# Routing inside the delta rule's walk, late zeroing of the experts' tails, and a wait per output bank in the last layer

## The reference

```python
for t in range(S):                                   # delta rule, 8 heads of 48, S = 768
    y[:, :, t] = einsum('bhd,bhde->bhe', q[:, :, t], state)
    v_old = einsum('bhde,bhd->bhe', state, kt)
    state = state + bt * einsum('bhd,bhe->bhde', kt, vt - v_old)
...
e_idx = argmax(x @ w_gate, axis=1)                   # 8 experts, one for each token
gate_w = probs[arange(N), e_idx]                     # softmax of the logits
eom = 1.0 / (1.0 + exp(-(x @ w_output_gate)))
for e in range(E):
    h = maximum(x[mask] @ w1[e], 0.0)                # 384 -> 1024
    out[mask] = gate_w[mask, None] * eom[mask, e, None] * (h @ w2[e])
...
h = maximum(maximum(x @ w1, x @ w2), x @ w3)         # 384 -> 768, three times
return h @ w_out                                     # 768 -> 384
```

## Time and profile before

| | |
|---|---|
| median of three runs | 1154.94 us (1149.84 to 1159.45) |
| profiled execution | 1154.56 us |
| its span in the trace | 1152.8 us |
| TensorE busy | 1012.1 us (88%) |
| VectorE busy | 482.1 us (42%) |
| ScalarE busy | 366.7 us (32%) |
| GpSimd busy | 324.4 us (28%) |

### The profile page before, as it was taken

How to read it: one execution, slowest core, us unless ns; L and a number is a source line. 1 busy time by engine, 2 the same in 40 slices (tenths; PEclk the granted TensorE clock), 3 DMA queues, 4 the chain that set the end, 5 groups by cost and what they waited for, 6 DMA issues and landing times. The chain is left out here.

```text
span 1152.8 us, 30762 instructions
## 1 busy us (share of the span) xinstructions
PE 1012.1 (88%) x13236; PEld 887.3 (77%) x13236; DVE 482.1 (42%) x922; ACT 366.7 (32%) x731; POOL 324.4 (28%) x226
## 2 busy tenths in 40 slices
PE   1789999999998999810899999999599999999999
PEld 1678878888887888710799999999578888888888
DVE  3455555555555554360344344344242314242321
ACT  0255545555554555410222222222121212122211
POOL 2232333233422421046545255453420101000000
PEclk9999999999999999955899999999889999999999
DMA  8712121220212100016324344432211000100000
GB/s 267 269 54 63 28 60 40 62 63 26 63 40 62 41 20 19 2 42 232 136 81 155 122 151 151 150 124 82 89 49 35 28 34 20 34 20 28 10 19 28
DMA packets 59394, 86.37 MB, mean 75 GB/s; under 512 B 29200, under 2 KB 54288, under 8 KB 56720
## 3 DMA queue, kind: packets, MB, share of 16 engines
q1 hardware_dynamic: 53616, 48.46, 13.1%
q0 software_dynamic: 5664, 36.18, 9.2%
HBM read 61.82 MB, written 22.81 MB: 73 GB/s over the span
## 5 line engine op out<-in xcount | busy, mean ns | idle before, releaser
L1029 PE MATMUL hb<-early,last_h 128*128 128x512 f32 x648 | 203.8, 396 | 4.7 <-ACT o_sb L1143 3.5
L1029 PEld LDWEIGHTS hb<-early,last_h 128*128 128x128 f32 x648 | 120.5, 189 | 30.8 <-ACT o_sb L1143 2.7
L1029 PE MATMUL hb<-early,last_l 128*128 128x512 f32 x324 | 126.9, 392 | 0.0
L480 DVE TENSOR_TENSOR p<-bank,cf 128x512 f16<-128x512 f32 x96 | 66.0, 688 | 45.1 <-PE bank L283 44.8
L283 PEld LDWEIGHTS bank<-t,n_hi 64*64 64x64 f16 x2688 | 66.2, 111 | 21.1 <-issue 5.7
L1167 DVE TENSOR_TENSOR m<-hb,m 128x512 f32<-128x512 f32 x36 | 24.9, 691 | 131.4 <-PE hb L1029 131.4
L283 PE MATMUL bank<-t,n_hi 64*64 64x64 f16 x2688 | 71.6, 195 | 4.6 <-issue 3.9
L1029 PE MATMUL ob<-wo_h,early 128*128 128x384 f32 x288 | 74.2, 335 | 0.0
L1029 PEld LDWEIGHTS hb<-early,last_l 128*128 128x128 f32 x324 | 61.3, 189 | 13.2
L951 POOL TENSOR_TENSOR late<-w_raw,late 128x3072 fp32r<-128x3072 f32 x8 | 54.4, 6801 | 56.3 <-DVE late L923 56.0
L585 POOL COPY x_all<-y_tile 128x384 f32<-128x384 f32 x24 | 12.1, 503 | 205.3 <-ACT y_tile L451 205.3
(11 more groups left out here) (155 smaller groups left out, 2191.4 us busy)
## 6 DMA issues: line engine op xcount, KB each, us to landing
w_raw<-w POOLq DMA_DIRECT2D x14, 1536.0 KB, 7.6
kq_t<-qh SPq DMA_DIRECT2D x24, 256.0 KB, 3.3
x_sorted<-zeros SPq DMA_DIRECT2D x32, 192.0 KB, 1.9
x_in<-x_sorted SPq DMA_DIRECT2D x29, 192.0 KB, 2.4
y_sorted<-y_sb SPq DMA_DIRECT2D x28, 192.0 KB, 1.9
k_raw<-kt_in SPq DMA_DIRECT2D x24, 192.0 KB, 3.5
k_own<-kh SPq DMA_DIRECT2D x24, 192.0 KB, 3.3
v_in<-vh SPq DMA_DIRECT2D x24, 192.0 KB, 3.3
```

Source lines behind the costliest of these rows:

```text
L480: dve.tensor_tensor(p16[st][:], pb, mask_of(lv), ALU.mult).then_inc(prod_out[st], 1)
L1029: ins = pe.matmul(out, a[x], b[y], start=first and i == 0, stop=last and i == 2, skip_group_check=True)
```

## The change

- Each tile is routed within the walk. After its logits VectorE finds the choice with four more operations, TensorE ranks it with two matmuls (`rank`, slot 15 of `CHAIN`) against a running count, VectorE works out the rows and raises the count (`slot`, 16), and GpSimd scatters the tile (`send`, 17). Each expert has an area of its own in `x_sorted`, with a fixed start, so that a row needs no total. `y_tile` is doubled. The order of the tiles within `CHAIN`'s part of a slot is turned round.
- The logits' matmuls have 16 columns; they had 128, of which 112 were padding.
- `x_sorted` is not zeroed at the start. The two tiles behind an expert's last row are zeroed when the count is known: the first expert's at the attention's end, the others' at the start of the expert before. Each expert gets two tiles at least (`MINB`). The tail of `y_sorted` is zeroed in pieces between Sync's loads.
- The first expert's weights are split in six pieces in six walks (`NORM` 10, 11, 12), and the second expert's are loaded from walk 9 on (13).
- `route_and_sort` is gone. Its table is made at the end of the attention part, its gates in the first tile of `experts`. Expert results are written three tiles further on in `y_sorted` (`LEAD`).
- In `last_layer` the wait for all four copies at a block's end is gone; each output bank has its own.

```diff
+MINB = 2
+MAXB = TILES + (E - 1) * MINB
...
-    CHAIN = {0: ("ks", 0), 2: ("z", 0), 4: ("up", 0), 6: ("ks", 1), 8: ("z", 1), 10: ("up", 1), 12: ("yt", 0), 14: ("lg", 0)}
-    NORM = {1: [0], 2: [1], 3: [2], 5: [3], 6: [4], 7: [5], 8: [6], 9: [7, 8], 10: [9]}
+    CHAIN = {0: ("ks", 0), 2: ("z", 0), 4: ("up", 0), 6: ("ks", 1), 8: ("z", 1), 10: ("up", 1), 12: ("yt", 0), 14: ("lg", 0),
+             15: ("rank", 0), 16: ("slot", 0), 17: ("send", 0)}
+    NORM = {1: [0], 2: [1], 3: [2], 4: [10], 5: [3], 6: [4], 7: [5], 8: [6], 9: [7, 8], 10: [9], 12: [11], 13: [13], 14: [12]}
...
-                for of, off in ((a, 0), (c, SLOTS), (b, 2 * SLOTS)):
+                for of, off in ((b, 2 * SLOTS), (c, SLOTS), (a, 0)):
...
-        with sp.Fori(0, MAXB + 1) as g:
-            sp.dma_start(xs[bass.ds(P * g, P), :], zeros[:]).then_inc(xs_zeroed, 16)
-
-        with sp.Fori(TILES, MAXB + 1) as g:
-            sp.dma_start(ys[bass.ds(P * g, P), :], zeros[:]).then_inc(xs_zeroed, 16)
...
+            for i in range(BLANK * (k - 2) // (STEPS - 2), BLANK * (k - 1) // (STEPS - 2)):
+                at = P * (LEAD + TILES + i)
+                sp.dma_start(ys[at:at + P, :], zeros[:]).then_inc(zeroed, 16)
+        sp.wait_ge(zeroed, 16 * BLANK)
+        sp.wait_ge(tabled, 8)
+        row = sp.value_load(table[0:1, 2, 0:1], min_val=0, max_val=N)
+        sp.dma_start(xs[bass.ds(row, MINB * P), :].rearrange("(n p) x -> p n x", p=P),
+                     zeros[:].unsqueeze(1).broadcast_to((P, MINB, X))).then_inc(zeroed, 16)
+        sp.wait_ge(zeroed, 16 * BLANK + 16)
...
-                    pe.wait_ge(logit_out[st], k)
+                    pe.wait_ge(routed[st], 5 * k - 1)
...
-                    ins = pe.matmul(out[:, X:X + P], y_t[st][:, c, :], wr[:, c, :], start=c == 0, stop=c == KX - 1,
+                    ins = pe.matmul(out[:, X:X + 2 * E], y_t[st][:, c, :], wr[:, c, :], start=c == 0, stop=c == KX - 1,
...
+            elif what == "rank":
+                pe.wait_ge(chosen_ready[st], k + 1)
+                if 2 * k + st >= 1:
+                    pe.wait_ge(counted_ready, 2 * k + st)
+                pe.sem_inc(passed_pe, 1)
+                pe.matmul(out[:, X + P - E:X + P], tri16, chosen[:, 2 * k + st, :], start=True, stop=False, skip_group_check=True)
+                pe.matmul(out[:, X + P - E:X + P], ones16, counted[:], start=False, stop=True,
+                          skip_group_check=True).then_inc(rank_done[st], 1)
...
+        pe.wait_ge(counted_ready, TILES)
+        pe.sem_inc(passed_pe, 1)
+        pe.matmul(bank[0][0][:, 0:E], ones16, counted[:], start=True, stop=True, skip_group_check=True).then_inc(totals_done, 1)
...
-                if e == 0 and k >= 1:
-                    act.wait_ge(x_out[st], k)
-                act.copy(y_tile[st][half[e], :], yb[st][C:P, 0:X]).then_inc(y_out[st], 1)
+                if e == 0 and k >= 2:
+                    act.wait_ge(rows_sent[st], 16 * (k - 1))
+                act.copy(y_tile[par][st][half[e], :], yb[st][C:P, 0:X]).then_inc(y_out[st], 1)
...
+                to = 2 * k + st
+                dve.tensor_copy(logits[:, to, :], yb[st][:, X:X + 2 * E]).then_inc(logit_out[st], 1)
+                dve.wait_ge(logit_out[st], k + 1)
+                dve.tensor_reduce(best[:, st:st + 1], logits[:, to, 0:E], AX.X, ALU.max).then_inc(routed[st], 1)
+                dve.wait_ge(routed[st], 5 * k + 1)
+                dve.scalar_tensor_tensor(out=score[st][:], in0=logits[:, to, 0:E], scalar=best[:, st:st + 1],
+                                         in1=cf[:, CF_IOTA:CF_IOTA + E], op0=ALU.is_equal, op1=ALU.mult).then_inc(routed[st], 1)
+                dve.wait_ge(routed[st], 5 * k + 2)
+                dve.tensor_reduce(top[:, st:st + 1], score[st][:], AX.X, ALU.max).then_inc(routed[st], 1)
+                dve.wait_ge(routed[st], 5 * k + 3)
+                dve.tensor_scalar(chosen[:, to, :], score[st][:], top[:, st:st + 1], None, ALU.is_equal).then_inc(chosen_ready[st], 1)
+            elif what == "slot":
+                to = 2 * k + st
+                dve.wait_ge(rank_done[st], k + 1)
+                dve.tensor_tensor(place[st][:], yb[st][:, X + P - E:X + P], chosen[:, to, :], ALU.mult).then_inc(routed[st], 1)
+                dve.wait_ge(routed[st], 5 * k + 4)
+                dve.tensor_reduce(slot_f[:, to:to + 1], place[st][:], AX.X, ALU.add).then_inc(routed[st], 1)
+                dve.wait_ge(routed[st], 5 * k + 5)
+                dve.tensor_copy(rows_at[:, to:to + 1], slot_f[:, to:to + 1]).then_inc(slot_ready[st], 1)
+                dve.tensor_tensor(counted[:], counted[:], chosen[:, to, :], ALU.add).then_inc(counted_ready, 1)
...
+            elif part in (10, 11, 12) and 2 <= k < 2 + PIECES:
+                if k == 2 and part == 10:
+                    for i in range(2):
+                        dve.wait_ge(weights.raw_in[i], 16)
+                cols = slice((k - 2) * KX * F // PIECES, (k - 1) * KX * F // PIECES)
+                i = part - 11
+                if part == 10:
+                    for raw, (hi, lo), ready in zip((0, 1), first_split, weights.hi_ready):
+                        ins = dve.tensor_copy(hi[:, cols], weights.flat_raw(raw)[:, cols])
+                        if k == 1 + PIECES:
+                            ins.then_inc(ready, 1)
+                        else:
+                            ins.then_inc(piece_done, 1)
...
+                    hi, lo = first_split[i]
+                    ins = dve.tensor_tensor(lo[:, cols], weights.flat_raw(i)[:, cols], hi[:, cols], ALU.subtract)
...
+        dve.wait_ge(totals_done, 1)
+        dve.tensor_tensor(more[:], bank[0][0][:, 0:E].unsqueeze(2).broadcast_to((P, E, TILES)),
+                          cf[:, CF_STEP:CF_STEP + E * TILES].rearrange("p (e t) -> p e t", e=E), ALU.is_gt).then_inc(tabled, 1)
+        dve.wait_ge(tabled, 1)
...
-            if what == "yt":
-                pool.wait_ge(y_out[st], 2 * k + 2)
-                pool.tensor_copy(x_all[:, 2 * k + st, :], y_tile[st][:]).then_inc(x_out[st], 1)
+            if what == "send":
+                to = 2 * k + st
+                pool.wait_ge(slot_ready[st], k + 1)
+                if k >= 1:
+                    pool.wait_ge(rows_sent[st], 16 * k)
+                pool.indirect_dma_start(xs, bass.IndirectOffsetOnAxis(ap=rows_at[:, to:to + 1], axis=0),
+                                        y_tile[par][st][:], None).then_inc(rows_sent[st], 16)
...
+            elif part == 13 and k == STEPS - 2:
+                for i, w in enumerate((w1, w2)):
+                    pool.wait_ge(weights.lo_ready[i], 1)
+                    pool.dma_start(weights.raw[i][:], w[1]).then_inc(weights.raw_again[i], 16)
...
-def route_and_sort(nc, ctx, sems, cf, x_all, logits, gate, slots, table, xs, xs_zeroed, weights, w1, w2):
...
+        def tile(e, g, off):
+            sp.wait_ge(xt_done, g)
+            sp.dma_start(x_in[:], xs[bass.ds(P * g + P * off, P), :]).then_inc(x_got, 16)
+            sp.wait_ge(y_out, g + 1)
+            sp.dma_start(ys[bass.ds(P * g, P), :], y_sb[:]).then_inc(y_sent, 16)
...
+            if e + 1 < E:
+                row = sp.value_load(table[0:1, 2, e + 1:e + 2], min_val=P * AREA * (e + 1), max_val=P * AREA * (e + 1) + N)
+                sp.dma_start(xs[bass.ds(row, MINB * P), :].rearrange("(n p) x -> p n x", p=P),
+                             zeros[:].unsqueeze(1).broadcast_to((P, MINB, X))).then_inc(zeroed, 16)
+            off = sp.value_load(table[0:1, 0, e:e + 1], min_val=0, max_val=AREA * e)
+            end = sp.value_load(table[0:1, 1, e:e + 1], min_val=MINB * (e + 1), max_val=MAXB)
+            with sp.Fori(begin, end) as g:
...
-        dve.memset(y_sb[:, 0:1], 0.0).then_inc(y_sent, 17)
-        dve.memset(y_sb[:, 1:2], 0.0).then_inc(y_out, 1)
...
+        dve.memset(y_sb[:], 0.0).then_inc(y_out, LEAD)
+        gates_first()
         split_x(0)
+        gates_last()
...
+            elif now is not None:
+                pe.wait_ge(o_out, NT * now + 1)
...
-                if t >= 2:
-                    pe.wait_ge(o_out, NT * n + t - 1)
+                pe.wait_ge(o_out, NT * n + t + 1)
...
-            pe.wait_ge(o_out, NT * n + NT)
```

322 lines of the change are left out of this document (149 added, 173 removed).

## The result

The changed kernel is slower. Its median is 1198.69 us (1195.44 to 1199.9, four executions), beside 1157.2 us (1149.84 to 1162.96, four) for the kernel before: ratio 1.036, with a 95% interval of 1.029 to 1.042. I had put 0.01 on that side. The profiled execution has a span of 1198.2 us against 1152.8, so it is 45.4 us that the two traces have to account for.

What follows compares the result with a forecast made beforehand. TensorE was taken to bound the kernel, with the routing the one large hole it doesn't fill. Hole -44, body +5, start -0.5 and last layer -3.6 sum to -43.1, from 1154.6 to 1111.5 us; range 1100 to 1125.

Steps and rivals of the forecast that it cites:

- The hole: Routing between attention and experts, where TensorE idles: 58.2 us would shrink to 14.3 with the last walk's share, -44.
- the last walk: End of attention: TensorE's ranking ahead of the state product adds 1.2 us, narrower last logits matmuls give back 0.5.
- The table's branch: After the last tile's slots: count, total, table, register load and zeroing, about 6.3 us; the scatter branch longer by some 0.5.
- The attention's body: Walks of the attention: TensorE -3 us, waits behind VectorE's added operations 8, net +5, between -8 and +16.
- six logits passes with 16 columns: TensorE in the attention: narrower logits matmuls would save 0.35 us per tile, 8 us in all.
- The choice's waits in the walks: At the second half's logits, ranking on TensorE waits for VectorE's four choice operations: 0.5 us a walk.
- The pieces at nothing: The 24 split pieces of the first expert's weights on VectorE in the walks cost nothing, 0.1 us each if not.
- the 0.5 at the start: Kernel start: constants for which GpSimd waits are 0.15 MB smaller, -0.5 us.
- Last layer: Dropping the wait for all four output copies saves 0.72 us at each of five block boundaries, -3.6 us.
- B: Rival: order of VectorE's small operations delays products in the attention's walks, +24 us there, whole 1131; chance 0.11.
- C: Rival: VectorE's split pieces in the walks wait for GpSimd's masks at the shared port, 23 us, whole 1133; chance 0.06.
- E: Rival: VectorE paces the attention, its added 51 us and 23 of port waits fully exposed, whole 1181; chance 0.02.

Runs made afterwards that it cites:

- other kernels without padding: Changed kernel with gram's stall removed by reordering and no bytes added behind the early weight tiles, in five variants; last logits copy 509.8 to 513.5 us.
- the 416 bytes: Changed kernel with GpSimd's scatter one slot later, plus 416 unused bytes per partition behind the early weight tiles; 1129.88 us, ratio 0.976 to the kernel before.
- send at slot 18: Changed kernel with GpSimd's scatter moved from slot 17 to 18, behind the other half's scaled keys; 1132.53 us, ratio 0.980 to the kernel before.
- choice after the walks: Changed kernel with choice, ranking and row numbers moved behind the last walk and no scatter; last logits copy 499.6 us, whole 1194.03 us.

## Why the prediction was wrong, by its steps

**The hole: right.** I had 13.6 us from the last logits copy to the first expert matmul, and it is 13.4. (The other 0.7 of the 14.3 was the last walk, which is below.) The rows of the changed kernel, to be laid beside the earlier trace rows:

```profile
580.45 0.17 DVE L549 COPY logits<-chain 128x16 f32<-128x16 f32 x1 [3.13 <-PE chain L443]
...
581.32 0.23 DVE L558 TENSOR_SCALAR chosen<-score,top 128x8 f16<-128x8 f32 x1
...
582.32 0.15 DVE L566 CAST rows_at<-slot_f 128x1 uint32<-128x1 f32 x1
...
582.75 0.97 POOL L698 DMA_INDIRECT x_sorted<-y_tile,rows_at  x1 [8.75 <-DVE rows_at L566]
...
584.94 0.17 DVE L664 CAST table<-shift 128x8 int32<-128x8 f32 x1
586.19 0.42 SPq L309 DMA_DIRECT2D x_sorted<-zeros  x1
589.10 0.34 SPq L804 DMA_DIRECT2D x_in<-x_sorted  x1
...
593.83 1.19 PE L779 MATMUL h_bank<-early,xt_h 128*128 128x512 f32 x2 [1.25 <-DVE xt_l L910]
```

Choice and slot take 2.02 us from the copy's start to the end of `rows_at` (I had 2.05), and the first load comes 8.65 us after the copy (9.05). One detail was the other way round: The scatter had been issued by 583.72, the zeroing whose address comes from the table only at 586.19, and Sync's last wait before the new stage (2.1 us) is for that zeroing. The table's branch is the longer one. The last 4.73 us were 4.55 in the sum.

**The attention's body: wrong, and this is the step that failed.** The text said of the scatter: "Its place is two slots away from the operations for which TensorE waits, and an engine with 11 of 36 us of work can bear 3 us each." Neither half answers the question. The scatter itself is issued in 1.0 us, less than the 3 that I allowed; what costs is that it can't start before `rows_at`, and that GpSimd had been 7.7 us ahead of TensorE, on which Sync's queue and with it `gram` depended. I counted slots between operations of TensorE, but not what stands behind the scatter in GpSimd's queue, nor who waits for that. The wait in GpSimd's queue stood at nothing in the sum, and it is 70.7 us.

**The body, the rest of it.** I had +5, between -8 and +16, and without the stall it was +16 (and up to +20 in the other kernels without padding), at the upper bound and over it. Mis-sized terms: six logits passes with 16 columns take 0.84 us in a row where 128 take 0.94, so 0.1 us saved per tile and not 0.35, 2.4 us in place of 8. The line that I drew through 96 and 128 columns doesn't go on below, and the traces show what stays: the six weight loads in front of these matmuls take 0.74 us in both kernels, since the weights there are the 128x128 tile of tokens, and only the other operand got narrower. The choice's waits in the walks were 0.3 to 0.4 us as forecast, but the drain's last walk lost 3.2 where I had 1.2 less 0.5. The pauses put down to issue I had not considered at all. The pieces at nothing: nothing shows against it, though only their length was tried.

**Start, experts.** The first logits copy came at 91.3 us (92.4 before), but among the unpadded kernels at 90.7 to 92.6, so the 0.5 at the start can't be told. The expert stage got 1.5 us longer against none forecast. The median of h_bank<-early,xt_h is 394 ns in the changed kernel, and 389 before and with the 416 bytes; but with the send at slot 18 it is 394 as well, and there the stage took 274.5 us, as before. So what the 1.5 us are stays open.

**Last layer: the mechanism right, the result not.** The waits went (3.5 us), and where the tiles lie as before the stretch is 4.9 us shorter. The forecast didn't look at the addresses.

**The rivals.** None was what happened. B, C and E all looked for the loss on VectorE. E had the right sign, by 74 us of VectorE's work laid bare; the measured loss in the attention was 86.7, by an engine that stood idle. What the text named as signs would have misled: "of 38 or more mean B" and "if the body is longer by more than 12 us, the placing on VectorE is what I misread" both lead to VectorE, and only the row of `gram` in the waits leads to GpSimd. (C's price was added up a little low: 22.7 us on top of 1111.5 is 1134 and not 1133.)

## What to carry to other kernels

When an operation that depends on the slowest engine's newest result is put into another engine's queue, ask how far that engine was ahead, list what stands behind the operation in its queue, and follow each of those to the next queue, until one arrives at the bottleneck. A low busy share says how much work an engine can take, not how long a wait in it can be borne. Place such an operation behind whatever frees a buffer for a load, even by one slot.

## What the runs showed of the hardware

TensorE's pace depends on where tiles lie in SBUF, the core's on-chip memory, and most likely on where its two operands lie. The same 128x512 matmuls took 392 to 393 ns with the last layer's weights a multiple of 512 bytes behind the early tiles, 397 with 128 over, 399 with 32 or 96 over, at one granted clock; that made 5.4 us in 266 in the kernel before, and 6.5 in the changed one. The distances are worked out from the tiles' widths, and why they matter no run says. The Trainium skill (SBUF — State Buffer, section Who interferes with whom) gives TensorE two independent read ports and says that it never waits on anyone. That section has nothing of addresses, so the 5.4 and 6.5 us here can't be read from it; whether the two reads get into each other's way is not shown.

A stall of 5.9 us costs more than itself: the 4.2 us behind it ran at 0.52 of the clock, and 32 matmuls took 3.68 us in place of 1.96. Shorter pauses sometimes had the lower clock behind them and sometimes not: behind 1.88 us (send at slot 18, 398.6) and 2.20 us (choice after the walks, 371.1) the clock was 0.66 and 0.63 over 4 us, behind 1.93 us (kernel before, 370.9) it stayed at 1.00.

A scatter's issue took 2.95 and 2.96 us while VectorE subtracted two tiles in SBUF (507.15 to 513.76), and 0.97 from the next one at 514.90 on (kernel before); in the walks of the changed kernel it took 1.02 on the average. In the other direction, in the changed kernel, a subtraction of 512 columns took 1.81 us in place of 0.68 beside GpSimd's multiplication. The same section of the Trainium skill has such an operation of VectorE contend with GpSimd's reads, and the second case agrees (1.81 us). It infers that such an operation would leave the issuing of transfers alone, and the first case doesn't bear that out (2.95 and 2.96 us against 0.97).
